# Attention and two MoE layers on one core: low parts, values, softmax sums and x splits moved within the attention pipeline

## The reference

```python
# B, H, S, D = 4, 8, 576, 64
scores = q @ k.T / sqrt(D) + bias[head]      # bias: 8 heads, from log distances
attn = exp(scores - max(scores))
attn = attn / (sum(attn) + 1e-09)
x = (attn @ v), heads side by side           # 2304 tokens x 512
h = x @ w_in                                 # 512 -> 2048
x = (s * relu(h)**2 + b) @ w_out             # 2048 -> 512
h = x @ w2_in
out = (h - tanh(h)) @ w2_out
```

## Time and profile before

| | |
|---|---|
| median of the runs | 1169.8 us |
| profiled execution, its own time | 1172.88 us |
| its span, first to last instruction | 1171.1 us |
| mean granted TensorE clock | 0.99 |
| TensorE busy | 1119.2 us (96%) |
| ScalarE (ACT) busy | 713.6 us (61%) |
| VectorE (DVE) busy | 620.2 us (53%) |
| GpSimd (POOL) busy | 603.8 us (52%) |
| DMA | 172.47 MB, mean 147 GB/s |

### The profile page before, as it was taken

One profiled execution on the slowest core, in us unless ns is written; L12 is line 12 of the kernel. 1 busy time (PEld: TensorE's weight loads), 2 busy tenths in 40 slices (PEclk: granted clock), 3 DMA queues, 4 the chain that ended last, 5 costly groups with the idle time before them and its releaser, 6 DMA issues.

```text
span 1171.1 us, 17786 instructions
## 1 busy us (share of the span) xinstructions
PE 1119.2 (96%) x6304; PEld 993.9 (85%) x6304; DVE 620.2 (53%) x1087; ACT 713.6 (61%) x1358; POOL 603.8 (52%) x511
## 2 busy tenths in 40 slices
PE   5677889999999999999999999999999999999998
PEld 1156778999999999999999999999888888999998
DVE  5967876744674276347653763575253163260440
ACT  8966776755776477557665765676365264472552
POOL 1035574656565556555654555554445445555553
PEclk9989999999999999999999999999999999999999
DMA  4677664455445534553465445442333333333332
GB/s 142 239 232 230 213 190 140 144 172 159 130 157 180 185 125 145 179 168 133 149 191 158 147 149 175 149 137 86 111 104 114 97 108 112 127 114 112 105 107 73
DMA packets 69753, 172.47 MB, mean 147 GB/s; under 512 B 8832, under 2 KB 15776, under 8 KB 69664
## 3 DMA queue, kind: packets, MB, share of 16 engines
q1 hardware_dynamic: 69376, 171.25, 46.0%
q10 hardware_dynamic: 288, 0.07, 0.0%
HBM read 155.59 MB, written 15.69 MB: 146 GB/s over the span
## 4 chain that ended last, share of the span: by engine, by line
PE 88%; ACT 5%; DMA 2%; DVE 2%; issue 1%; POOL 1%; SPq 0%; ACTq 0%; DVEq 0%; POOLq 0%
PE ps_f L677 23%; PE ps_f L675 23%; PE ps_f L676 23%; PE ps_t L465 6%; PE ps_o L435 3%; PE ps_s L454 3%; PE ps_o L437 3%; PE ps_s L455 3%; ACT x_raw L305 2%; ACT w_raw L322 1%; DMA inv_rows<-inv_row 1%; DVE p_t L563 1%; DVE ptl L582 1%; PE ps_f L465 1%; DMA inv_b<-inv_rows 0%
## 5 line engine op out<-in xcount | busy, mean ns | idle before, releaser
L632 POOL TENSOR_TENSOR wl<-w_raw,wh 128x512 fp32r<-128x512 f32 x320 | 417.8, 1311 | 442.6 <-ACT wh L625 442.4
L675 PE MATMUL ps_f<-xh,wh 128*128 128x464 f32 (+1 forms) x640 | 239.0, 373 | 2.4 <-DVE ptl L582 2.4
L677 PE MATMUL ps_f<-xh,wl 128*128 128x464 f32 (+1 forms) x640 | 238.2, 372 | 0.0
L675 PE MATMUL ps_f<-gh,wh 128*128 128x464 f32 (+1 forms) x640 | 238.0, 372 | 0.0
L677 PE MATMUL ps_f<-gh,wl 128*128 128x464 f32 (+1 forms) x640 | 237.6, 371 | 0.0
L676 PE MATMUL ps_f<-xl,wh 128*128 128x464 f32 (+1 forms) x640 | 237.6, 371 | 0.0
L676 PE MATMUL ps_f<-gl,wh 128*128 128x464 f32 (+1 forms) x640 | 237.1, 370 | 0.0
L625 ACT ACTIVATE wh<-w_raw 128x512 fp32r<-128x512 f32 x320 | 197.9, 623 | 45.5 <-PE ps_f L677 45.3
L563 DVE CUSTOM_DVE_ANT_0 p_t<-ps_s,bias_t 128x576 f32<-128x576 f32 x158 | 118.4, 750 | 102.5 <-PE ps_s L455 97.6
L509 ACT ACTIVATE p_t<-p_t,neg_max 128x576 f32<-128x576 f32 x160 | 124.1, 775 | 62.1 <-DVE neg_max L563 61.7
L698 ACT ACTIVATE r_buf<-ps_f 128x464 f32<-128x464 f32 (+1 forms) x160 | 89.1, 557 | 113.1 <-PE ps_f L677 113.1
(11 more groups left out here) (78 smaller groups left out, 1542.0 us busy)
## 6 DMA issues: line engine op xcount, KB each, us to landing
w_raw<-in_w_in SPq DMA_DIRECT2D x80, 512.0 KB, 3.7
w_raw<-in_w_out SPq DMA_DIRECT2D x80, 512.0 KB, 3.7
bias_t<-bias_flat SPq DMA_DIRECT2D x128, 288.0 KB, 2.8
bias_flat<-w_raw SPq DMA_DIRECT2D x36, 295.5 KB, 2.2
q_raw<-in_qt SPq DMA_DIRECT2D x32, 288.0 KB, 3.2
k_raw<-in_kt SPq DMA_DIRECT2D x32, 288.0 KB, 4.2
v_raw<-in_vt SPq DMA_DIRECT2D x32, 160.0 KB, 2.9
bias_t<-bias_flat SPq DMA_DIRECT2D x32, 144.0 KB, 3.0
```

The source lines that it names most:

```text
L632: pool.tensor_tensor(wl[:, b % RING, :, :], raw_block(b), wh[:, b % RING, :, :].bitcast(F32), ALU.subtract).then_inc(w_lo_done, 1)
L675: pe.matmul(acc, hi, rhs_h[:, k0 + kk, 0:T], start=(first and kk == 0), stop=False)
L677: mm = pe.matmul(acc, lo, rhs_h[:, k0 + kk, 0:T], start=False, stop=(last and kk == 3))
```

## The change

- Tiles are counted through all heads (`g`, `i`), and a step is one number `g`. Values run two steps behind the turn instead of one (`valued(g)` = g - 7, `turned(g)` = g - 5). The list of steps is one longer.
- TensorE's order in a step is scores, values, turn; at t = 2, where a head's values begin, scores, turn, values.
- In the alone stage the low part `ptl` is made one step after its turn (`dve_low(turned(g - alone))`), and one more call after the last alone step; the first block now waits for tile 42's low part instead of tile 43's.
- In the alone stage ScalarE does the exponential of tile 4 ahead of `pth`.
- The last key tile is stacked: its low part goes to partitions 64 to 127 of `pth` (`low_home`), v's padding rows hold the 64 keys a second time, and the tile's values take one matmul per column half.
- The sums are turned (`pe_turn_den`, at t = 3 ahead of the scores) in place of their reciprocals. VectorE adds 1e-9 as it reads them from PSUM into `inv_row` and takes the reciprocal there, on 5 x 128, after the low part. `den_e` and `inv` are gone.
- GpSimd scales x and makes q's low part at t = 1 (were t = 0 and t = 2); all four x splits of unit 0 are on GpSimd, the fourth right after the scaling of head 7 in step (9, 1).
- SyncE stores the inverse sums before it loads q and k, loads v of head n at (n, 0) instead of (n-1, 4), and loads the last bias tile of head 0 ahead of the steps.

The diff, cut to its core:

```diff
@@ -51,7 +52,8 @@
     bias_skew = bias_flat[1:1 + S * (H * PITCH - 1)].rearrange("(i w) -> i w", w=H * PITCH - 1)
 
 
-    STEPS_AT = [(s // NT, s % NT) for s in range((BH + 1) * NT + 1)]
+    TILES = BH * NT
+    STEPS_AT = list(range(TILES + NT + 2))
     FIRST = (H + 1) * NT + 1 + EXTRA
     PLACES = ([1, 3, 5, 7, 9, 11, 13] + [16, 17, 18, 19, 20, 21, 22, 24, 25, 26, 27, 28, 29, 30] +
...
@@ -396,17 +395,22 @@
 
         inv_rows = nc.dram_tensor("inv_rows", (BH, NT * P), F32, kind="Internal").ap()
 
-        def slot(n, t):
-
-            return (n * NT + t) % 2
+        def slot(i):
+
+            return i % 2
 
         def score_bank(n, t):
 
             return ps_o if n == 0 and t % 2 else ps_s
 
-        def turn_bank(n, t, alone):
-
-            return flat(ps_f if alone and slot(n, t) else ps_t)
+        def low_home(i):
+
+            R = ROWS[i % NT]
+            return pth[P - R:P, slot(i), :] if R < P else ptl[:, slot(i), :]
+
+        def turn_bank(i, alone):
+
+            return flat(ps_t if i % 2 or not alone else ps_f)
 
...
@@ -425,17 +429,27 @@
             else:
                 eng.wait_ge(y_done, u * KD + i - KF + 1)
 
-        def pe_value(pe, n, u):
-            pe.wait_ge(pt_lo_done, n * NT + u + 1)
+        def turned(g):
+
+            return g - NT if 0 <= g - NT < TILES else None
+
+        def valued(g):
+
+            return g - NT - 2 if 0 <= g - NT - 2 < TILES else None
+
+        def pe_value(pe, i):
+            n, u = divmod(i, NT)
+            pe.wait_ge(pt_lo_done, i + 1)
             if u == 0:
                 pe.wait_ge(v_lo_done, n + 1)
                 need(pe, o_done, n)
             for half in range(2):
                 cols = slice(half * HALF, (half + 1) * HALF)
-                pe.matmul(ps_o[:, half, 0:HALF], vhl[:, n % 2, u, :], pth[:, slot(n, u), cols],
-                          start=(u == 0), stop=False)
-                mm = pe.matmul(ps_o[:, half, 0:HALF], vhl[:, n % 2, u, :], ptl[:, slot(n, u), cols],
-                               start=False, stop=(u == NT - 1))
+                mm = pe.matmul(ps_o[:, half, 0:HALF], vhl[:, n % 2, u, :], pth[:, slot(i), cols],
+                               start=(u == 0), stop=(u == NT - 1))
+                if u < NT - 1:
+                    mm = pe.matmul(ps_o[:, half, 0:HALF], vhl[:, n % 2, u, :], ptl[:, slot(i), cols],
+                                   start=False, stop=False)
             mm.then_inc(pv_done, 1)
 
         def pe_score(pe, n, t):
...
@@ -455,69 +469,78 @@
                 mm = pe.matmul(acc, lhs, k2l[:, n % 2, cols], start=False, stop=True)
             mm.then_inc(s_done, 1)
 
-        def pe_turn(pe, v, t, alone):
+        def pe_turn(pe, i, alone):
+            v, t = divmod(i, NT)
             if t == 0:
                 pe.wait_ge(exp_done, (v + 1) * NT)
-            need(pe, pt_lo_done, v * NT + t - alone)
+            need(pe, pt_lo_done, i - alone)
             R = ROWS[t]
-            acc = turn_bank(v, t, alone)
-            for i in range(NT):
-                mm = pe.transpose(acc[0:R, P * i:P * (i + 1)], p_t[:, v % 2, i, P * t:P * t + R], ident[:])
+            acc = turn_bank(i, alone)
+            for r in range(NT):
+                mm = pe.transpose(acc[0:R, P * r:P * (r + 1)], p_t[:, v % 2, r, P * t:P * t + R], ident[:])
             mm.then_inc(pt_done, 1)
 
-        def pe_turn_inv(pe, v):
-            pe.wait_ge(inv_done, v + 1)
-            need(pe, inv_row_done, v)
+        def pe_turn_den(pe, v):
+            pe.wait_ge(exp_done, (v + 1) * NT)
+            need(pe, den_done, v)
             if scoring(v + 1):
                 pe.wait_ge(min_done, (v + 1) * NT + 3)
-            pe.transpose(ps_s[0:NT, 0, HALF:HALF + P], inv[:], ident[:]).then_inc(inv_turned, 1)
-
-        def pe_step(pe, n, t, alone):
-
-            v = n - 1
-            if t and turning(n):
-                pe_turn(pe, v, t, alone)
+            pe.transpose(ps_s[0:NT, 0, HALF:HALF + P], den[:, v % 2, :], ident[:]).then_inc(den_turned, 1)
+
+        def pe_step(pe, g, alone):
+
+            n, t = divmod(g, NT)
             if t == 3 and turning(n):
-                pe_turn_inv(pe, v)
+                pe_turn_den(pe, n - 1)
             if scoring(n):
                 pe_score(pe, n, t)
...
-            if turning(n):
+            if valued(g) is not None and t != 2:
+                pe_value(pe, valued(g))
+            if turned(g) is not None:
+                pe_turn(pe, turned(g), alone)
+            if valued(g) is not None and t == 2:
+                pe_value(pe, valued(g))
+
+        def act_step(act, g, alone, between=None):
+            n, t = divmod(g, NT)
+            i, j = turned(g), valued(g)
+
+            def exponential():
                 if t == 0:
-                    pe_turn(pe, v, 0, alone)
-                else:
-                    pe_value(pe, v, t - 1)
-
-        def act_step(act, n, t, alone, between=None):
-            if t == 0 and n >= 2:
-                act.wait_ge(pv_done, (n - 2) * NT + NT)
+                    need(act, den_turned, n - 1)
+                act.wait_ge(min_done, g + 1)
+                p = p_t[:, n % 2, t, :]
+                act.activation(p, p, ACT.Exp, scale=-1.0, bias=neg_max[:, t:t + 1],
+                               accum_out=den[:, n % 2, t:t + 1]).then_inc(exp_done, 1)
+
+            if j is not None and j % NT == NT - 1:
+                act.wait_ge(pv_done, j + 1)
                 act.activation(o_tmp[:], ps_o[D:P, :, 0:HALF], ACT.Copy).then_inc(o_low_done, 1)
-            if turning(n):
-                v, R = n - 1, ROWS[t]
-                act.wait_ge(pt_done, v * NT + t + 1)
-                need(act, pv_done, v * NT + t - 1)
-                act.activation(pth[0:R, slot(v, t), :], turn_bank(v, t, alone)[0:R, 0:S], ACT.Copy)\
+            if scoring(n) and alone and t == NT - 1:
+                exponential()
+            if i is not None:
+                R = ROWS[i % NT]
+                act.wait_ge(pt_done, i + 1)
+                need(act, pv_done, i - 1)
+                act.activation(pth[0:R, slot(i), :], turn_bank(i, alone)[0:R, 0:S], ACT.Copy)\
                     .then_inc(pt_hi_done, 1)
             if between:
                 between()
-            if scoring(n):
-                if t == 0:
-                    need(act, den_done, n - 1)
-                act.wait_ge(min_done, n * NT + t + 1)
-                p = p_t[:, n % 2, t, :]
-                act.activation(p, p, ACT.Exp, scale=-1.0, bias=neg_max[:, t:t + 1],
-                               accum_out=den[:, n % 2, t:t + 1]).then_inc(exp_done, 1)
+            if scoring(n) and not (alone and t == NT - 1):
+                exponential()
             if t == 1 and n + 1 < BH:
                 act_round_q(act, n + 1)
 
-        def pool_step(pool, n, t):
+        def pool_step(pool, g):
+            n, t = divmod(g, NT)
             if t == 0 and n + 1 < BH:
                 pool_round_k(pool, n + 1)
                 pool_low_k(pool, n + 1)
-            if t == 0 and n >= 2 and n % 2 == 1:
+            if t == 1 and n >= 2 and n % 2 == 1:
                 pool_scale(pool, n - 2)
-            if t == 2 and n + 1 < BH:
+                if n == H + 1:
+                    pool_split(pool, KD - 1)
+            if t == 1 and n + 1 < BH:
                 pool_low_q(pool, n + 1)
             if t == 3 and scoring(n):
                 pool.wait_ge(v_loaded, (n + 1) * DMA)
...
@@ -548,14 +571,23 @@
             at = h // H * S % RINGX
             return x_raw[rows, h % H // 2, at:at + S]
 
-        def dve_step(dve, n, t, alone, between=None):
+        def dve_low(dve, i, alone):
+            R = ROWS[i % NT]
+            dve.wait_ge(pt_hi_done, i + 1)
+            dve.tensor_tensor(low_home(i), turn_bank(i, alone)[0:R, 0:S], pth[0:R, slot(i), :].bitcast(F32),
+                              ALU.subtract).then_inc(pt_lo_done, 1)
+
+        def dve_step(dve, g, alone, between=None):
+
+            n, t = divmod(g, NT)
+            i, j = turned(g - alone), valued(g)
             if scoring(n):
-                dve.wait_ge(s_done, n * NT + t + 1)
+                dve.wait_ge(s_done, g + 1)
             if t == 3 and turning(n):
                 v = n - 1
-                dve.wait_ge(inv_turned, v + 1)
+                dve.wait_ge(den_turned, v + 1)
                 need(dve, inv_stored, v * DMA)
-                dve.tensor_copy(inv_row[:], ps_s[0:NT, 0, HALF:HALF + P]).then_inc(inv_row_done, 1)
+                dve.tensor_scalar(inv_row[:], ps_s[0:NT, 0, HALF:HALF + P], 1e-9, None, ALU.add).then_inc(den_done, 1)
             if scoring(n):
                 dve.wait_ge(bias_loaded[t], (n + 1) * DMA)
                 if t == 0:
@@ -564,38 +596,32 @@
                                          in1=halves(bias_t[:, t, :]), scale=-SCALE, scalar=3.0e38,
                                          op0=ALU.add, op1=ALU.min, accum_out=neg_max[:, t:t + 1])\
                     .then_inc(min_done, 1)
```

(67 more changed lines are left out.)

37 lines of the change are left out of this document (16 added, 21 removed).

## The result

The changed kernel takes 1150.9 us (median of four runs, 1149.9 to 1152.6) against 1169.8: a ratio of 0.984, with a 95% interval of 0.982 to 0.986. That is 18.9 us less; 14.0 were forecast.

A forecast was written before the change was run, and what follows sets the result against it. TensorE's own work bounds the mixed stage, the order of head steps the alone stage. Savings of 4.0 (mixed), 8.4 (alone) and 1.6 (clock) make 14.0 us: 1169.8 to 1155.8 us, range 1148.5 to 1163.5.

The forecast's parts named there:

- main forecast: Whole kernel: median becomes 1155.8 us, bracket 1151 to 1160, chance 0.60.
- rival 2: Alone stage: q and k loads land a us sooner, odd heads also take 9.8; 7.1 us more won, 1149, chance 0.12.
- the 14.0 us of the sum: Whole kernel: 4.0 us from the mixed stage, 8.4 from the alone stage, 1.6 from the clock at the first block.
- mixed stage: Attention steps beside MoE blocks: 44 fewer value matmuls save 5.9 us, less 1.9, net 4.0 (2.5 to 5.9).
- the 1.9 us for turning the sums apart: Mixed stage, t = 3: sums turned apart from other transpositions make one more change per head, 24 x 0.08 us lost.
- the single bank: Mixed stage: with one bank `ps_t` a turn waits for the low part of the one before; costed at nothing.
- GpSimd's wait at t = 1: Mixed stage: GpSimd waits for ScalarE's rounded q, weights' low parts queue behind; 7.6 us of cover, costed at nothing.
- rival 4: Mixed stage: GpSimd delays weights past their cover, TensorE stops in each of 24 heads; 24 us longer, 1194, chance 0.04.
- The free head: Alone stage: a head not held by loads takes 8.75 + 0.3 + 0.1 + 0.6 = 9.75 us, against 11.6 before.
- list of signs: Expected trace: 424 value matmuls, 1.75 us in steps 0 and 4, 0.9 us reciprocal, first block near 169.5.
- The load loop: Alone stage, heads 3, 5, 7: next q and k loads wait for GpSimd's low q, so 11.2 us each.
- The first block: First MoE block: starts 8.2 us into head 9 after a 0.9 us wait, without half clock, saving 1.6 us.

The follow-up runs named there:

- the two partial versions: Changed kernel with only low parts back in their turn's step: 1172.0 us; with lags and TensorE's order undone, VectorE's and ScalarE's orders kept: 1174.0 us.

## Why the prediction was right, and where it was not

The measured 1150.9 us lies in the stated range, but 0.1 us below the bracket of the main forecast (1151 to 1160) and nearer to rival 2 (1149) than to 1155.8. Against the 14.0 us of the sum the spans differ by 20.3: 4.0 more in the alone stage, 1.6 more in the mixed stage, and 0.7 ahead of head 1.

**The mixed stage.** The count of 44 matmuls and their price were right: 424 in the trace, 0.133 us each by the unstacked kernel (with the 0.13 that the prediction writes the product is 5.7, with 0.133 it is its 5.9). The term that was wrong is the 1.9 us for turning the sums apart from the other transpositions. The step with the turned sums, from its first instruction to the second matmul of the next block, takes 1.93 us both before and after, in one such step as in the mean of all 22. First the rows of the kernel before, then those of the changed kernel:

```profile
241.96 0.71 PE L465 MATMUL ps_t<-ident,p_t 128*128 128x128 f32 x5
242.51 0.27 PE L473 MATMUL ps_s<-ident,inv 128*5 128x128 f32 x1
...
243.89 0.37 PE L676 MATMUL ps_f<-gl,wh 128*128 128x464 f32 x1
...
196.24 0.27 PE L488 MATMUL ps_s<-ident,den 128*5 128x128 f32 x1
196.27 0.38 PE L468 MATMUL ps_s<-k2h,q 128*128 128x288 f32 x1
...
197.87 0.46 PE L701 MATMUL ps_f<-xh,wh 128*128 128x464 f32 x1
198.17 0.37 PE L702 MATMUL ps_f<-xl,wh 128*128 128x464 f32 x1
```

The transposition of the sums takes a slot of 0.03 us. The second change that the prediction priced is there after (0.38 and 0.46 instead of 0.29 and 0.37), but before, the turn with the small transposition behind it took 0.55 us and not the 0.46 of a turn alone: that price was already paid. So the value was near the upper bound, 5.9: 7.2 for the stage less 1.6 for the clock is 5.6.

**No waits in the mixed stage.** Right: the list of waits behind the first block is empty. Neither the single bank nor GpSimd's wait at t = 1 costs anything, and rival 4 did not happen.

**The free head.** 9.75 forecast, 9.7 to 9.9 measured. The places inside were partly others, and part of the agreement is luck: steps 1 and 2 together take 4.12 where the sum had 3.80, and the other three are 0.07, 0.03 and 0.11 under theirs. Step 1 is 1.63, and it is step 2 (2.49) that the sum of the halves delays, as the next minimum stands behind it (head 5):

```profile
120.85 0.75 DVE L608 TENSOR_TENSOR x_raw<-ps_o,o_tmp 64x576 f32<-64x576 f32 x1
121.63 0.76 DVE L595 CUSTOM_DVE_ANT_0 p_t<-ps_s,bias_t 128x576 f32<-128x576 f32 x1
```

The reciprocal delays step 4 (2.24 against 1.76 with it on 5 columns: 0.5, forecast 0.6); the prediction's list of signs, which has 1.75 us for steps 0 and 4, had forgotten that. The one wait left for a low part (0.9 us, in head 3) lies behind the late load there.

**The reciprocal.** 0.90 forecast from two widths, 0.93 measured at 5 x 128, which is 0.74 more than on 5 columns, or 6.0 ns for each of the 123 between them. The estimate of 1.2 us from the Trainium skill ("VectorE: DVE Perf Modes", the fixed hardware budget) is too long; the measurement decides.

**The load loop, the step that failed.** The prediction said of GpSimd's instructions in the odd heads that their order does not change, and so took 11.2 us for each of them. The order does change: `pool_scale` and `pool_low_q` now stand together in step 1 of `pool_step`, and `pool_split` is called behind it. That takes 1.8 us out of the chain, and k lands sooner besides, 3.9 us after its issue in head 5 instead of 4.3 (3.8 for 4.8 in the means above). Heads 5 and 7 took 9.9. The stage came to 91.6 where the sum had 95.6. Head by head the sum had 11.2, 9.8, 12.9, 11.0, 11.2, 9.8, 11.2, 10.3 and 8.2; against the table above heads 5 and 7 hold 2.7 of the 4.0, head 3 0.7 and head 1 0.4, and the other five are within 0.1. So in heads 5 and 7 what happened is rival 2, which had 0.12, partly for the reason that it named (loads that land a us sooner) and partly for one that it did not (the order on GpSimd). Of the 7.1 us that rival 2 gave, 3.4 came: head 3 with its late load and head 4 with its fall of the clock took 12.2 and 11.0, near the 12.9 and 11.0 of the forecast. The start of head 1, 0.7 us earlier here, was not in the sum, and its cause is not shown: over all runs that point lies at 73.1 to 73.8 with the last bias tile loaded as before, and at 72.3 to 74.2 with it loaded ahead of the steps.

**The first block.** 1.6 us of clock forecast, and 1.6 is what the mixed stage loses when the fourth split goes back. Head 9 8.2 forecast, 8.3 measured; the wait is 0.6 for 0.9.

**What the schedule is worth.** The forecast gave the waits of 8.9 us to the two lags. It said that the addition of 1e-9 lay in the chain of every head, from one row of 1.35 us; but in the nine heads of the kernel before it took 1.04, 1.41, 0.17, 0.66, 1.35, 0.17, 0.17, 0.31 and 1.18 us. The experiments split the gain otherwise: the schedule of before reaches 10.0 us a head where the addition is short or gone, and 10.4 with the long reciprocal (its step 4 takes 2.24 instead of 1.75); the lags bring it to 9.8. So a free head went from 11.2 (with the addition held by GpSimd) to 10.0 without it, up to 10.4 by the long reciprocal, and down to 9.8 by the lags. The forecast had the right end, 9.8, and the wrong shares: it gave the lags most of the way. Taken out of the changed kernel one by one, the stacked tile is worth 8.0 us by the medians, the fourth split 5.9, the lags 5.3 and low q ahead of the split 4.6; what the rows of the traces show of each is 6.4, 4.3, 4.8 and 2.4.

## What to carry to other kernels

Write down the order of each in-order queue from the code of both versions, call by call, before costing a loop: here the place of one call on GpSimd was worth 4.5 us to the kernel before, a quarter of what the change gained. When a stall is removed and the time stays, look for the wait that grew by the same amount; taking the addition of 1e-9 out alone changed nothing that could be measured, while the waits for GpSimd grew. And undo or move a schedule as one piece: the order on three engines and the lag go together, since the two partial versions that were run were 21 and 23 us slower than the whole.

## What the runs showed of the hardware

The reciprocal on VectorE grows with its width at about 6 ns a column (0.191, 0.370 and 0.93 us for 5, 36 and 128), about five times the 1.2 ns a column of the low part beside it (0.67 us from start to start for 576). The number of partitions doesn't show: 640 sums take 0.93 us as 5 x 128 and 0.19 as 128 x 5.

The addition of 1e-9 on VectorE, 128 x 5 from SBUF to SBUF, took 0.17 us in 9 of the 32 heads of the kernel before. In the other 23 it began during an instruction of GpSimd and ended 0.02 to 0.03 us behind it, as from 89.76 to 91.17 beside a subtraction from 89.72 to 91.15. Where it began just ahead (137.12, GpSimd's next at 137.21) it was not held. The same addition reading PSUM, in the changed kernel, took 0.27 to 0.28 us in all 32 heads, 29 of them with GpSimd at work.

And whether the clock falls after a short wait differs between executions. In head 3 of the changed kernel's profile TensorE waited 0.93 us for a low part and then 1.48 us for low q, the granted clock fell to 0.54 (106 to 108), and head 4 took 11.0 us. The kernel with the reciprocal on 5 columns had the same two waits (0.90 and 1.48), the clock stayed at 1.00, and head 4 took 9.2.
